# The low parts of the rows of three products move from GpSimd to VectorE in an attention and gated-convolution kernel

## The reference

```
scores = q k^T / 8 + slope[h] * -|i - j|,  only for 0 <= i - j < 128
x   = softmax(scores) v                      -> (4, 576, 512)
h   = relu(x @ w_in)                         -> (4, 576, 1024)
g1  = h * sigmoid(conv over the sequence, 3 taps, of h)
x2  = g1 @ w_out                             -> (4, 576, 512)
val = x2 @ w_val
g2  = val * sigmoid(causal conv over the sequence, 5 taps, of x2)
y   = g2 @ w_out2                            -> (4, 576, 512)
```

## Time and profile before

| | |
|---|---|
| median of 3 runs | 513.11 us (511.14 to 514.45) |
| the profiled execution | 511.86 us |
| its span in the profile | 509.9 us |
| mean granted clock of TensorE | 0.956 |
| busy: TensorE, VectorE, ScalarE, GpSimd | 453.4, 382.4, 259.9, 152.8 us |

### The profile page before, as it was taken

The page is one execution under the profiler, slowest core; times in us unless marked ns, Lnnn a source line. Parts: engine busy times, 40 slices in busy tenths (PEclk is TensorE's granted clock), DMA queues, the critical chain, the costliest instruction groups (busy, mean ns, idle before and its releaser), DMA issues.

```text
span 509.9 us, 9587 instructions
## 1 busy us (share of the span) xinstructions
PE 453.4 (89%) x3424; PEld 421.6 (83%) x3424; DVE 382.4 (75%) x1080; ACT 259.9 (51%) x756; POOL 152.8 (30%) x178
## 2 busy tenths in 40 slices
PE   2777836969799999999899999999799999999996
PEld 2557736869688998899788998899688998898996
DVE  4896988789778498759678498749788498759730
ACT  2365453335655547544656557445655647355231
POOL 4750556424311044104311044104311044104520
PEclk9899958879899999999799999999899999999998
DMA  8457100100121101220021101220121100010011
GB/s 215 138 156 269 41 3 21 42 21 12 31 63 42 59 2 41 64 68 17 26 64 42 58 1 43 63 68 11 33 63 42 59 1 1 1 48 0 1 48 46
DMA packets 38927, 25.80 MB, mean 51 GB/s; under 512 B 22752, under 2 KB 35040, under 8 KB 38880
## 3 DMA queue, kind: packets, MB, share of 16 engines
q1 hardware_dynamic: 38880, 25.20, 17.0%
HBM read 20.47 MB, written 4.72 MB: 49 GB/s over the span
## 4 chain that ended last, share of the span: by engine, by line
PE 53%; DVE 33%; issue 6%; ACT 5%; SPq 1%; DMA 1%; POOLq 0%; POOL 0%; DVEq 0%
DVE conv L543 13%; PE bank L658 11%; PE bank L659 11%; PE bank L660 11%; PE bank L607 7%; PE bank L621 7%; PE bank L642 6%; DVE conv L550 5%; DVE conv L538 4%; DVE gate L570 3%; DVE probs L512 2%; DVE guarded L505 2%; ACT L431 2%; DVE gate L557 2%; DMA taps<-taps 1%
## 5 line engine op out<-in xcount | busy, mean ns | idle before, releaser
L658 PE MATMUL bank<-g_hi,w_hi 128*128 128x288 f32 x384 | 123.6, 322 | 5.5 <-POOL g_lo L326 1.9
L658 PE MATMUL bank<-x_hi,w_hi 128*128 128x290 f32 (+1 forms) x384 | 116.1, 302 | 6.6 <-DVE x_lo L527 6.6
L659 PE MATMUL bank<-x_lo,w_hi 128*128 128x290 f32 (+1 forms) x384 | 115.1, 300 | 0.0
L659 PE MATMUL bank<-g_lo,w_hi 128*128 128x288 f32 x384 | 114.8, 299 | 0.0
L660 PE MATMUL bank<-g_hi,w_lo 128*128 128x288 f32 x384 | 114.8, 299 | 0.0
L660 PE MATMUL bank<-x_hi,w_lo 128*128 128x290 f32 (+1 forms) x384 | 114.6, 299 | 0.0
L326 POOL TENSOR_TENSOR g_lo<-conv,g_hi 128x288 fp32r<-128x288 f32 x64 | 56.0, 881 | 168.0 <-ACT g_hi L421 168.0
L543 DVE SCALAR_TENSOR_TENSOR conv<-hidden,taps,conv 128x288 f32<-128x288 f32 x128 | 88.9, 695 | 4.5
L387 ACT COPY probs_t<-bank 128x512 f32<-128x512 f32 (+1 forms) x80 | 40.1, 502 | 83.4 <-PE bank L621 83.4
L570 DVE SCALAR_TENSOR_TENSOR gate<-x_all,taps,gate 128x288 f32<-128x288 f32 x128 | 78.6, 614 | 4.5
L658 PEld LDWEIGHTS bank<-g_hi,w_hi 128*128 128x128 f32 x384 | 73.9, 192 | 7.8 <-DVE gate L557 2.9
(11 more groups left out here) (46 smaller groups left out, 575.8 us busy)
## 6 DMA issues: line engine op xcount, KB each, us to landing
w_raw<-panels SPq DMA_DIRECT2D x12, 512.0 KB, 5.8
y_t<-y_sb SPq DMA_DIRECT2D x32, 144.0 KB, 1.8
q_tile<-q_t SPq DMA_DIRECT2D x32, 128.0 KB, 2.9
k_all<-k_t SPq DMA_DIRECT2D x16, 256.0 KB, 3.4
v_tile<-v_tiles SPq DMA_DIRECT2D x16, 256.0 KB, 2.6
q_tile<-q_t SPq DMA_DIRECT2D x8, 64.0 KB, 2.5
k_all<-k_t SPq DMA_DIRECT2D x4, 128.0 KB, 2.7
v_tile<-v_tiles SPq DMA_DIRECT2D x4, 128.0 KB, 2.9
```

The costliest lines, as they stand in the source:

```text
L658: pe.matmul(out, w_hi[:, p, col:col + P], hi(k), start=start, stop=False)
L659: pe.matmul(out, w_hi[:, p, col:col + P], lo(k), start=False, stop=False)
```

## The change

The three helpers `g1_low`, `g2_low` and `x2_low` move from GpSimd's program to VectorE's, with the same operands, the same waits and the same semaphores; only the engine differs. `g2_low` comes one beat earlier than it did on GpSimd. GpSimd keeps the weight panels and the four columns of history. VectorE's beat begins with `g1_low(c, j-2)`, then `tap_rows(c, j)` and `gated(c, j-1)`; `g2_low(c-1, j-VAL0-1)` stands behind `val_rows`, and `x2_low` ahead of `conv2_rows`. The panels stand on GpSimd at the same beats, which it reaches without the low parts between them.

```diff
 @block.gpsimd
-            def g1_low(c, m): ...   def g2_low(c, m): ...   def x2_low(c, m): ...
             def beat(c, j):
-                if c < CHUNKS and 2 <= j < KW + 2:
-                    g1_low(c, j - 2)
-                if c > 0 and 0 <= j - VAL0 - 2 < KM:
-                    g2_low(c - 1, j - VAL0 - 2)
                 if c < CHUNKS and j == VAL0 + 3:
                     keep_history(c)
-                if c < CHUNKS and j >= DOWN0 + 2 and j < DOWN0 + 2 + 2 * KM and j % 2 == 0:
-                    x2_low(c, (j - DOWN0 - 2) // 2)
 @block.vector
+            def g1_low(c, m):
+                n = KW * c + m
+                dve.wait_ge(g1_hi_done, n + 1)
+                dve.tensor_tensor(g1_lo[:, m, :], conv[n % DEPTH][:, :], g1_hi[:, m, :],
+                                   ALU.subtract).then_inc(g1_lo_done, 1)
+            def g2_low(c, m):
+                dve.wait_ge(g2_hi_done, KM * c + m + 1)
+                dve.tensor_tensor(g2_lo[:, m, :], gate2[:, m, :], g2_hi[:, m, :],
+                                   ALU.subtract).then_inc(g2_lo_done, 1)
+            def x2_low(c, m):
+                dve.wait_ge(x2_hi_done, KM * c + m + 1)
+                dve.tensor_tensor(x2_lo[:, m, :], x2_all[:, m, LEFT:LEFT + HALF], x2_hi[:, m, :],
+                                   ALU.subtract).then_inc(x2_lo_done, 1)
             def beat(c, j):
+                if c < CHUNKS and 2 <= j < KW + 2:
+                    g1_low(c, j - 2)
                 if c < CHUNKS and j < KW:
                     tap_rows(c, j)
                 if c < CHUNKS and 1 <= j < KW + 1:
                     gated(c, j - 1)
                 if c > 0 and 0 <= j - VAL0 < KM:
                     val_rows(c - 1, j - VAL0)
+                if c > 0 and 0 <= j - VAL0 - 1 < KM:
+                    g2_low(c - 1, j - VAL0 - 1)
                 if c < CHUNKS and DOWN0 + 2 <= j <= OUT0 and j % 2 == 0:
+                    x2_low(c, (j - DOWN0 - 2) // 2)
                     conv2_rows(c, (j - DOWN0 - 2) // 2)
```

More of the change, by code:

```diff
@@ L321, in split_panel @@
                                    ALU.subtract).then_inc(w_split, 1)
[L323 to L337, removed]
             def keep_history(c):
```

## The result

The changed kernel takes 545.67 us (median of 3 runs, 543.78 to 548.53) against 513.11: slower, ratio 1.066, 95% interval 1.057 to 1.075. The span of the profiled execution grew from 509.9 to 543.7 us, by 33.8 us. In the new listing the lines moved: VectorE's multiply-adds are L521 and L548 (they were L543 and L570), `gated` L528, `val_rows` L535, and the low parts `g1_low` L556, `g2_low` L561, `x2_low` L566; on ScalarE the relu is L385, the sigmoid L391, the cast `g1_high` L399.

What follows compares the result with a forecast made beforehand. TensorE was the nominal bound (89% busy), with VectorE's row stage equally on the path. Even chunks 16.9, odd 13.3, chunk 7 6.2, chunk 0 0.3 and tail -0.4 gave +36.3 us on 511.86: 548 us, range 530 to 561.

Steps and rivals of the forecast that it cites:

- The new wait: Row stage, chunks 1 to 7: VectorE's g1_low stands 0.49 us for ScalarE's cast, row 2.71 us, +4.24 us a chunk.
- even chunks: Behind row stages of chunks 2, 4, 6: low parts queued ahead of normalise +0.9 us, TensorE clock dip +0.5 us each.
- Odd chunks: Behind row stages of chunks 1, 3, 5: longer TensorE pause before mix, clock dip costs 0.2 us more each.
- Chunk 7: Last chunk, where only down follows the row stage: half-clock time lost in full, 2.0 us.
- the tail: Final chain: the last low part is quicker on VectorE, saving 0.4 us; a milder clock dip might give 1.5 more.
- Chunk 0: First chunk: early weight panels and the cast wait add 11 us to the row stage; 10.7 us return behind it.
- The relief: VectorE multiply-adds without GpSimd's interference: a pair back from 1.49 to 1.07 us, 0.42 us a row, 25 us busy time.
- That TensorE covers 19 us of a row stage: Row stage: TensorE's 12 products of 1.6 us level with VectorE at 19 us, so at most 2 of 4.24 us hide.
- the rival of no change: Row stage's added time hidden by TensorE's own products, so nothing to measure; chance 0.03.
- The rival of the clock: TensorE at half clock behind every row stage, 13 us more, 561 us in all; chance 0.15.
- The absorbed rival: Chunk 0 gains up to 10 us and later stages give back 1 to 2 us a chunk: 526 us; chance 0.15.
- The faster rival: Cast already done when VectorE comes, standstill under 0.05 us a row: row 2.14 us, 501 us in all; chance 0.03.

Runs made afterwards that it cites:

- e1: Changed kernel with g1_low moved from the start to the end of VectorE's beat, same subtractions: 510.91 us, ratio 0.9965 to the kernel before.
- e5: Changed kernel with g1_low between tap_rows and gated, and g2_low later in all but the last chunk: 499.34 us, ratio 0.9736 to the kernel before.
- e4: Kernel before plus only VectorE's wait for the g1_high cast at the start of the beat, subtractions still on GpSimd: 561.29 us, ratio 1.0956.
- e9: Changed kernel with 288-column filler matmuls on TensorE ahead of down (chunks 2, 4, 6, 7) and mix (chunks 1, 3, 5): 535.9 us, ratio 1.0474.
- e6: Changed kernel with GpSimd's panels 6 to 11 of chunk 0 held by waits to their old moments: 554.24 us, ratio 1.0826 to the kernel before.
- e3: Changed kernel with g1_low back on GpSimd, so only g2_low and x2_low move to VectorE: 511.81 us, ratio 0.9977 to the kernel before.
- e7: Kernel of e5 plus six extra 256-column subtractions a chunk on VectorE, with no wait of their own: 519.92 us, ratio 1.0149 to the kernel before.
- e8: Changed kernel with 30 filler matmuls of 64 columns on TensorE ahead of down in chunks 2, 4, 6 and 7: 546.33 us, ratio 1.0664.

## Why the prediction was right

The mechanism came out as said, and so did most of its size. The sum was 36.3 us, and the profiled spans differ by 33.8. Some of the closeness is luck: the terms missed by -0.7 (the wait), +1.5 (even chunks), +0.3 (odd), -2.0 (chunk 7) and -1.8 us (chunk 0), partly in opposite directions.

*The new wait, +4.24 us a chunk.* Measured 4.16 to 4.23 in chunks 2 to 7 and 3.85 in chunk 1, 29.0 against 29.7 for the seven. The standstill is 0.50 us where 0.49 was said, 0.80 in the first two rows, and a row 2.72 against 2.71. e1 and e5 show that it is the place, and e4 that a wait there slows the rows without any work, though with a collision of its own.

*Behind the row stage, even chunks, 0.9 for the queue and 0.5 for the clock.* The queue is 33.8 less 32.9, 1.0 us, in e9 where the clock stays up (chunk 6: 1.2). This is near the 0.9 said, but the path is not quite the one said: the first `normalise` comes 1.7 us later after the last `gated` than before (3.07 against 1.37 in chunk 2), and then the last `g2_low`, whose wait the sum put at nothing, stands still for 1.09 us in the change as in e1. Yet without that standstill, in e5, the stretch is only 0.2 us shorter, so it was nearly free; how 1.0 us comes of these delays stays open. The clock adds 1.4, 0.0 and 1.1. Together 5.7 against the 4.2 of the sum. That a half-clock stretch mostly hides beside the later VectorE was so in chunk 4 alone, where it lasted 3.4 us; in chunks 2 and 6 it lasted 6.8.

*Odd chunks, 0.2 each.* Measured 0.5, 0.1 and 0.4.

*Chunk 7, 2.0 for the clock, and 0.4 off in the tail.* Together +1.6 in the sum, -0.4 measured. The dip behind its row stage cost 1.5 (against e9), but the kernel before had a dip at its very end, worth 1.5 of the 1.9 us by which its end is longer than e9's, and that one is gone; the text named it as what "might give 1.5 more" and left it out of the sum.

*Chunk 0, +11 and -10.7.* Measured +9.5 and -11.3. e6 separates the panels from the wait: 5.8 us of the row stage were the early panels where 8.4 less 1 were said, and 3.7 the wait where 3.6 were said; 10.1 came back.

*The relief.* Here the working was mis-sized. "382 + 57 (128 x 0.45) - 25 (relief)" gives 414; VectorE's busy time is 388. Two things make up the difference. The subtractions do come to 58.5 us, but each overlaps its neighbours; the 0.37 us of issue time that the same prediction used, 47 us in all, would have been the figure to add. And the relief is 45.9 us where 25 were said: 17.1 in the multiply-adds of the rows, the only ones counted (20.0 outside chunk 0, less 2.9 that the early panels took there), 12.2 in `conv2_rows` and 16.6 in `normalise`, which were left out. It did not move the forecast, as e3 shows: it has most of that relief (68.4 us for `conv2_rows`, 44.4 for the multiplication of `normalise`, none in the rows), and its time is that of the kernel before.

*That TensorE covers 19 us of a row stage* was used against the rival of no change; e7 shows that it covers nothing there, since `down` waits for `val_rows` and `turn` for `normalise`, both queued behind the last row on VectorE.

The rival of the clock was wrong in its size (3 to 4 us net, not 17). The absorbed rival wanted 10 us from chunk 0 and 1 to 2 us from each later stage; chunk 0 gave 1.7, and no later stage but the end of chunk 7 (0.4) gave any. The faster rival named the point on which it turned, a standstill under 0.05 us a row; e5 reaches it, and 499 us is what its 501 became (6.4 us from the rows where it had 4, and 7.3 from chunk 0 where it had 6).

## What to carry to other kernels

When an instruction moves to another engine, price its place in the new queue before its duration: find what released it before, and look whether that releaser can have finished when the new engine comes to it. A low part that follows its own engine's product by way of a cast on another engine needs one row's work between them, and the instruction right ahead should not be the one whose semaphore the next one waits for. An engine that waits for free today pays for the same wait once it is the engine that sets the pace.

## What the runs showed of the hardware

A wait for a semaphore that the instruction right ahead on the same engine raises costs VectorE 0.19 us, though nothing else is late: from start to start 0.56 us in e1, against 0.38 for the same two instructions in the change, where the semaphore was raised by an older one (247.62 and 248.00), and 0.37 in e5.

GpSimd's subtraction held a multiplication with a single input for its whole length, 1.01 us for 0.36 (e4), more than it held back a pair of multiply-adds of which the first was under way, 1.49 for 1.07. The Trainium skill, "SBUF — State Buffer", section Who interferes with whom, says that where a VectorE instruction takes the ports that it shares with GpSimd, whoever issues first has them for the whole instruction and the other blocks in full. The trace agrees on the full blocking, since GpSimd's end, 253.03 + 0.80 = 253.83, lies just ahead of the multiplication's end at 254.00. It does not show that GpSimd was first: the multiplication is recorded from 252.99, 0.04 us ahead of it. The example that the prediction gave for two SBUF inputs (59.00 and 59.17) is of this kind too, a multiplication with a single input.

TensorE counted as busy for 3.70 of 3.70 us with matmuls of 64 columns (e8, chunk 2), and the clock still fell to 0.50 right behind them; with the same filling in chunk 4 it stayed at 1.00, and in chunks 2 and 6 it was down for 3.4 us where it is 6.8 in the change. With matmuls of 288 columns in these pauses and in those of the odd chunks (e9) it stayed at 1.00 for 449 us. What decides between the two stays open.
